# One-hot rows written token by token, and a copy of x moved from GpSimd to a DMA of SyncE

## What is computed

```python
# 1. attention in windows: chunks of 32 queries, 16 keys to the left, 8 to the right, 8 memory keys
# 2. experts
skip_score = x @ w_skip
do_compute = skip_score > 0
out = x.copy()
xc = x[do_compute]
logits = xc @ w_gate                       # 8 experts
e_idx = np.argmax(logits, axis=1)
gate_w = softmax(logits)[.., e_idx]
for e in range(E):
    mask = e_idx == e
    h = np.maximum(xc[mask] @ w1[e], 0.0)  # 512 -> 1024
    y[mask] = gate_w[mask, None] * (h @ w2[e])
out[do_compute] = xc + y
# 3. h = max(x @ w1, x @ w2, x @ w3); result = h @ w_out
```

## Time and profile before

| | us |
|---|---|
| three runs: median | 673.62 |
| lowest, highest | 672.19, 688.42 |
| the profiled execution's own time | 675.65 |
| its span, first to last instruction | 673.9 |
| PE busy in the span | 651.8 (97%) |
| DVE / ACT / POOL busy | 460.1 / 318.9 / 174.6 |
| granted TensorE clock, mean | 1.000 of full |

### The profile page before, as it was taken

One profiled execution on the slowest core, in us unless ns is written; L12 is line 12 of the kernel. 1 busy time (PEld: TensorE's weight loads), 2 busy tenths in 40 slices (PEclk: granted clock), 3 DMA queues, 4 the chain that ended last, 5 costly groups with the idle time before them and its releaser, 6 DMA issues.

```text
span 673.9 us, 13069 instructions
## 1 busy us (share of the span) xinstructions
PE 651.8 (97%) x4864; PEld 542.4 (80%) x4864; DVE 460.1 (68%) x820; ACT 318.9 (47%) x504; POOL 174.6 (26%) x210
## 2 busy tenths in 40 slices
PE   4999989999999999999999999999999999999998
PEld 3778865788997999988888888888888888888886
DVE  4778867877666656798899873378889516888500
ACT  4445442556544555564455453345456424445311
POOL 7411222476675375405300012100000220000000
DMA  8999964767675587713601115121101111110011
GB/s 301 410 328 341 344 232 175 262 233 265 199 245 166 180 298 248 234 41 119 214 32 63 62 48 188 47 64 62 63 32 63 59 67 52 44 63 32 0 63 62
DMA packets 32505, 101.07 MB, mean 150 GB/s; under 512 B 6012, under 2 KB 6156, under 8 KB 32336
## 3 DMA queue, kind: packets, MB, share of 16 engines
q1 hardware_dynamic: 26288, 87.12, 37.6%
q0 software_dynamic: 6176, 13.41, 5.7%
HBM read 87.11 MB, written 16.80 MB: 154 GB/s over the span
## 4 chain that ended last, share of the span: by engine, by line
PE 89%; DVE 4%; DMA 2%; issue 2%; ACT 1%; another core or an unknown queue 1%; SPq 1%; DVEq 0%; ACTq 0%
PE ps_c L1620 9%; PE ps_c L1622 9%; PE ps_c L1621 8%; PE ps_b L1622 5%; PE ps_b L1620 5%; PE ps_b L1621 5%; PE ps_s L1490 4%; PE ps_h L1620 4%; PE ps_h L1622 4%; PE ps_h L1621 4%; PE ps_o L1505 4%; PE ps_y L1620 3%; PE ps_y L1621 3%; PE ps_y L1622 3%; PE ps_f L1622 2%; PE ps_f L1620 2%
## 5 line engine op out<-in xcount | busy, mean ns | idle before, releaser
L1215 DVE TENSOR_TENSOR w_lo<-raw,w_hi 128x1024 fp32r<-128x1024 f32 x64 | 79.5, 1254 | 42.1 <-ACT w_hi L837 33.7
L837 ACT ACTIVATE w_hi<-raw 128x1024 fp32r<-128x1024 f32 x64 | 67.8, 1060 | 47.6 <-PE ps_y L1622 26.2
L1238 DVE TENSOR_TENSOR u_lo<-u_f,u_hi 128x1792 fp32r<-128x1792 f32 x27 | 54.6, 2023 | 50.3 <-ACT u_hi L826 50.3
L1620 PE MATMUL ps_c<-c_hi,u_lo 128*128 128x512 f32 x216 | 85.2, 394 | 0.6
L1622 PE MATMUL ps_c<-c_hi,u_hi 128*128 128x512 f32 x216 | 84.2, 390 | 0.0
L1621 PE MATMUL ps_c<-c_lo,u_hi 128*128 128x512 f32 x216 | 84.2, 390 | 0.0
L1620 PE MATMUL ps_h<-x_hi,w_lo 128*128 128x256 f32 (+1 forms) x256 | 71.5, 279 | 1.7 <-DVE w_lo L1215 0.9
L1622 PE MATMUL ps_h<-x_hi,w_hi 128*128 128x256 f32 (+1 forms) x256 | 71.9, 281 | 0.0
L1621 PE MATMUL ps_h<-x_lo,w_hi 128*128 128x256 f32 (+1 forms) x256 | 71.9, 281 | 0.0
L777 POOL DMA_INDIRECT out<-f_out,order x16 | 17.6, 1100 | 207.5 <-ACT f_out L792 206.9
L792 ACT ACTIVATE f_u<-ps_c 128x512 f32<-128x512 f32 x58 | 34.6, 597 | 69.8 <-PE ps_c L1622 67.5
(11 more groups left out here) (240 smaller groups left out, 1504.3 us busy)
## 6 DMA issues: line engine op xcount, KB each, us to landing
raw<-wpack SPq DMA_DIRECT2D x64, 512.0 KB
u_f<-wunit SPq DMA_DIRECT2D x27, 512.0 KB, 3.3
v_sb<-vW SPq DMA_DIRECT2D x32, 390.0 KB, 5.3
k_sb<-kT SPq DMA_DIRECT2D x32, 250.0 KB, 4.9
q_sb<-qT SPq DMA_DIRECT2D x16, 384.0 KB, 6.0
x_dram<-x_buf SPq DMA_DIRECT2D x4, 1536.0 KB, 10.2
f_in<-x_dram SPq DMA_DIRECT2D x1, 2048.0 KB, 9.0
out<-f_out SPq DMA_DIRECT2D x8, 256.0 KB, 2.0
```

The source lines that it names most:

```text
L837: act.activation(w_hi[c % RING][:, :], raw[:, c % RAW, :], ACT.Copy).then_inc(s_whi, 1)
L1215: dve.tensor_tensor(w_lo[c % RING][:, :], raw[:, c % RAW, :], w_hi[c % RING][:, :].bitcast(F32), ALU.subtract).then_inc(s_wlo, 1)
L1238: dve.tensor_tensor(u_lo[n % UBUF][:, 1:8, :], u_f[n % UBUF][:, 1:8, :], u_hi[n % 2][:, :, :].bitcast(F32), ALU.subtract).then_inc(s_ulo, 1)
L1620: pe.matmul(out_, a_lo, b_hi, start=first, stop=False, skip_group_check=goes_on)
```

## The change

`oh_row` is laid out token by token: `[P, NTT, P]`, so that the 128 numbers which PE loads for one column lie next to each other. It is written by 24 instructions in place of four: each compares the numbers 0 to 127 (`iota`, now stored once, not six times) with one number per partition, `row[:, t:t + 1]`, which is float32 instead of bfloat16. PE waits before each of its 24 products instead of before every sixth.

The copy of `x_in` to `x_nat` leaves GpSimd. SP starts a DMA for it in every pass (`keep_rows`), between the weight chunks 5 and 6, after it has waited for the gathered rows and for the sums of the pass before. GpSimd's next gather into `x_in` and DVE's sums wait for that DMA (`s_xnat`).

```diff
-            iota = sb("iota", [P, P, ROWS], BF16)
+            iota = sb("iota", [P, P], BF16)
-            row = sb("row", [P, NTT], BF16)
-            oh_row = sb("oh_row", [P, NTT // ROWS, P, ROWS], BF16)
+            row = sb("row", [P, NTT])
+            oh_row = sb("oh_row", [P, NTT, P], BF16)
...
+            def keep_rows(i):
+                for t in range(TB):
+                    sp.wait_ge(s_gath[t], i * 16 + 16)
+                sp.wait_ge(s_xo, i * TB + TB)
+                sp.dma_start(x_nat[:, :, :], x_in[:, :, :]).then_inc(s_xnat, 16)
+
+            def load_rest(e, i):
+                for c in range(LEAD, FB):
+                    load_chunk(e, c, i * FB + c + 1)
+                    if c == 5:
+                        keep_rows(i)
...
-                pool.iota(iota[:, :, :], pattern=[[1, P], [0, ROWS]], base=0, channel_multiplier=0,
+                pool.iota(iota[:, :], pattern=[[1, P]], base=0, channel_multiplier=0,
...
-            def take_rows(i):
-                pool.wait_ge(s_xo, i * TB + TB)
-                order_()
-                pool.tensor_copy(x_nat[:, :, :], x_in[:, :, :]).then_inc(s_nat, 1)
-
             def next_rows(i):
                 pool.wait_ge(s_tr, i + 1)
-                pool.wait_ge(s_nat, i * 2 + 1)
+                pool.wait_ge(s_xnat, i * 16 + 16)
                 pool.wait_ge(s_idx, i + 1)
...
-            for n in range(NTT // ROWS):
-                dve.tensor_tensor(oh_row[:, n, :, :], iota[:, :, :],
-                                  row[:, n * ROWS:(n + 1) * ROWS].unsqueeze(1).to_broadcast([P, P, ROWS]), ALU.is_equal)\
-                    .then_inc(s_row, 1)
+            for t in range(NTT):
+                dve.tensor_scalar(oh_row[:, t, :], iota[:, :], row[:, t:t + 1], None, ALU.is_equal).then_inc(s_row, 1)
...
             def sums_out(i, tokens):
-                dve.wait_ge(s_nat, i * 2 + 2)
+                dve.wait_ge(s_xnat, i * 16 + 16)
+                dve.wait_ge(s_nat, i + 1)
                 dve.wait_ge(s_landed, i + 1)
...
             for t in range(NTT):
-                n, j = t // ROWS, t % ROWS
-                if j == 0:
-                    pe.wait_ge(s_row, n + 1)
-                last = pe.matmul(spots, oh_row[:, n, :, j], val[:, :, :, t].rearrange("p v n -> p (v n)"),
+                pe.wait_ge(s_row, t + 1)
+                last = pe.matmul(spots, oh_row[:, t, :], val[:, :, :, t].rearrange("p v n -> p (v n)"),
                                  start=False, stop=(t == NTT - 1))
```

More of the change, by code:

```diff
@@ L77 @@
 B12, B11, B22, B21, T1, T2, T3, T4 = range(8)
-ROWS = 6
 NIX = 2
@@ L368, in build @@
         s_nat = sem("s_nat")
+        s_xnat = sem("s_xnat")
         s_h = sem("s_h")
@@ L496, in load_pass @@
                 e_next = sp.value_load(table[0:1, bass.ds(i + 1, 1)], min_val=0, max_val=E - 1)
-                for c in range(LEAD, FB):
-                    load_chunk(e_now, c, i * FB + c + 1)
+                load_rest(e_now, i)
                 for c in range(LEAD):
@@ L509, in _ @@
             e_last = sp.value_load(table[0:1, bass.ds(last, 1)], min_val=0, max_val=E - 1)
-            for c in range(LEAD, FB):
-                load_chunk(e_last, c, last * FB + c + 1)
+            load_rest(e_last, last)
             for n in range(2, UBUF):
@@ L681, in next_gates @@
                 pool.tensor_copy(idx_q[:, :], gidx[:, bass.ds(i * TB + TB, TB)]).then_inc(s_idxq, 1)
-                pool.wait_ge(s_nat, i * 2 + 2)
+                pool.wait_ge(s_nat, i + 1)
                 pool.wait_ge(s_idxq, i + 2)
@@ L718, in begin @@
             def begin(i):
-                take_rows(i)
                 next_rows(i)
@@ L724, in begin @@
                 rows_there(i - 1)
-            for t in range(TB):
-                pool.wait_ge(s_gath[t], 16)
-            take_rows(0)
             next_rows(0)
```

## The result

| | before | after |
|---|---|---|
| median of 22 runs each, us | 673.59 | 676.22 |
| lowest, highest | 671.83, 688.42 | 673.05, 679.43 |
| the profiled execution | 675.65 | 679.01 |
| its span | 673.9 | 676.9 |

The changed kernel is slower by 0.41%: ratio 1.0041, 95% interval [1.0028, 1.0054].

What follows compares the result with a forecast made beforehand. PE, busy 97% of the span, was taken to bound the kernel. One-hot rows +1.0 us and the x copy off GpSimd -1.1 us summed to -0.1 us: 673.5 us from the median 673.62, range 671.0 to 677.0.

Steps and rivals of the forecast that it cites:

- DVE's rate: Routing, one-hot rows: 24 DVE instructions start 0.20 us apart and become PE's clock, so `idx_f` comes 1.0 us later.
- The bounds of 0.13 and 0.27: Routing: limits for DVE's row spacing in us, putting `idx_f` between 0.6 us earlier and 2.7 us later.
- The middle: Routing: the chosen row spacing of 0.20 us between those limits, the rate of the instruction replaced.
- Rival 1: Routing: DVE rows cheaper, 0.16 us apart, costing +0.2 us; sum -0.9, total 672.7 us; chance 25%.
- The 20 added waits of PE lie within DVE's 0.20.: Routing, PE's 24 products: the extra waits add nothing beyond DVE's 0.20 us per row.
- The copy off GpSimd, -1.1 us: Pass 1: without GpSimd's copy the `w_lo` pair ends 1.2 us earlier and PE regains 0.9 to 1.2 us.
- SP's queue and the DMA engines: Start of passes: the x copy's DMA fits SP's spare 3 us and largely idle DMA engines; cost nothing.
- the hole: Pass 1, 142 to 144 us: DMA engines almost idle (0.05 and 0.00), where the x copy would largely fall.
- my upper bound of 6.1: The 512 KB x copy by DMA: bounded between 3.3 and 6.1 us.
- GpSimd's chain ... Both still fit ... Nothing.: Passes 0 and 1: gather 1.6 to 4.4 us later, yet `g_nat` and `rows_there` still in time; cost nothing.
- Rival 3: Passes 0 and 1: x copy delays chunk 6 or 7 by over 1 us; +1.9, 675.5 us; chance 18%.
- rival 4: Pass 3: ACT's unexplained 2.98 us pause goes or another comes, giving 670.8 or 676.3 us; chance 10%.

Runs made afterwards that it cites:

- experiment 1: Kernel before with only the new one-hot rows (`oh_row`), GpSimd still copying x: 677.15 us, ratio 1.0022.
- 4: Kernel before with the new one-hot rows and PE reading its two loop bounds ahead of the 24 products: 674.71 us, ratio 1.0011.
- experiment 14: Kernel before with GpSimd gathering the gates of pass 0 before it takes the rows: 673.88 us, ratio 0.9996.
- experiment 12: Kernel before plus an unused 512 KB SBUF-to-SBUF DMA per pass but the last, in SP's queue where the change copies x: 674.28 us, ratio 1.0006.
- 13: Changed kernel with PE's two reads ahead of the 24 products and GpSimd gathering pass 0's gates before waiting for the copy: 673.18 us, ratio 0.9978.
- 5: Changed kernel with the x copy of pass 0 started behind weight chunk 3 instead of chunk 5: 675.4 us, ratio 1.0014.
- 8: Changed kernel with GpSimd gathering the gates of pass 0 before it waits for the x copy: 677.23 us, ratio 1.0029.
- experiment 15: Changed kernel, unedited, profiled a second time: 674.01 us.
- experiment 3: Changed kernel with PE reading its two loop bounds before the 24 products instead of after them: 679.23 us, ratio 1.0052.

## Why the prediction was wrong

The time moved by +0.41% where the sum gave -0.1 us. By its own steps:

- **DVE's rate.** The step took 0.20 us a row and `idx_f` +1.0 us. Measured: 0.163 us and +0.2 us. The bounds of 0.13 and 0.27 held it. The middle was too high: either the number per partition and the width don't cost one after the other as I had added them, or the width costs less in this form; the runs don't tell the two apart. By the Trainium skill ("VectorE: DVE Perf Modes", section on the perf-mode tier table) `tensor_scalar` on bfloat16 in SBUF runs at twice the rate of `tensor_tensor`; with the fixed part from the earlier trace rows that gives, as an estimate, starts 0.16 us apart, and the trace agrees with its 0.163. Rival 1 had this step right.
- **"The 20 added waits of PE lie within DVE's 0.20."** This step failed first. They do, each for itself; but I counted the waits and not what stands behind the last. Before, the last row was done at 111.97, 2.0 us before the filling began at 113.96, and the reads fitted in between, or so the absence of any gap says; now the last row is done at 113.83, the reads come after it, and PE stands still for 1.22 us. Experiments 1 and 4 show it by taking the reads away. By itself the pause would have cost little, since before PE waited 1.33 us for the first rows anyway; nor did slow filling products by themselves, as experiment 14 shows. The two together, a start 1.6 us later and 1.7 us more of filling, are more than that slack: the rows landed 0.8 us later, PE turned them 1.0 us after that, and less the 0.25 us that it used to wait for `x_lo` this is the +1.5 us to the first product. That the pause made the clock fall isn't shown. All six profiles with the pause have slow filling products (5.96 to 7.36 us), but so have three of the five with the new rows and the reads ahead (5.55, 5.61 and 6.18), and one of the seven with the old rows (experiment 14).
- **The copy off GpSimd, -1.1 us.** Near in size, but partly by luck in place. In the changed kernel the pair of `w_lo` takes 2.35 us and PE's pause is gone, as said. But that pause belongs to the one execution before that I had read. Of the other four with GpSimd's copy, experiment 1 has a pair of 2.99 us and a pause of 0.37, and 4, 12 and 14 have 2.35 to 2.42 and no pause. There the copy held up DVE in pass 0 instead: `u_f` took 1.14 and 1.26 us (4, 12) in place of 0.42, and `moved` 1.79 (14), where 4 has 0.19. So most of the 1.55 us that 13 wins in pass 1 is not the copy's: 4, with the copy on GpSimd, has a pass 1 of 17.77, and 13 has 17.68. The nearest pair is 4 and 13, both with the new rows and the reads ahead: 13 is 0.8 us shorter up to the end of pass 1, nearly all of it before the first product, and the two ratios, on two chips, are apart (1.0011 [0.9999, 1.0023] and 0.9978 [0.9962, 0.9995]).
- **SP's queue and the DMA engines.** The copy didn't fall into the hole alone but in pass 0 behind three chunks, and took 6.45 us, just beyond my upper bound of 6.1. The traffic itself costs nothing that can be measured (experiment 12), as the step said.
- **"GpSimd's chain ... Both still fit ... Nothing."** The second failure, and the larger one. The shift was forecast well: gather at 125.0 to 127.8 (measured 127.79), gates later by 1.6 to 4.4 us. I then checked two of the things that hang on the chain, `g_nat` and `rows_there`. `g_nat` came 6.6 us later, since each gather on the way took up to 1.1 us longer; it cost 0.4 us in pass 0. I didn't check the third, the gather of pass 1, against PE's turn of the rows in step 6 of that pass. It moved from the hole at 142 to 144 us into the busiest stretch of the DMA engines, and PE waited 3.9 us for it, or ACT for chunks. Experiments 5 and 8 show it from two sides: either one brings the gather back to about 145.5, and the waits are gone in its profile. Rival 3 had the place (GpSimd's chain, the chunks) and near the size (675.5), at 18%, but a chunk late by over 1 us, which it wanted, is in only one of the three profiles (experiment 15).
- **The pause in pass 3** went away, rival 4's good end, and this hid 2.9 us of the loss in the profile. (Its 2.98 us on either side of 673.5 give 670.5 and 676.5, not the 670.8 and 676.3 written there; nothing hangs on it.) Pauses of 1 to 3 us without a cause that the trace shows stand in passes 2 to 4 of several kernels, the kernel before among them, and in others not.

What stays open: what makes the clock fall during the filling products; why the half clock holds for 20 us and more in some executions once it is there; what ends up late in pass 1 of a given execution; and whether the pauses of passes 2 to 4 have to do with any of these edits.

## What to carry to other kernels

When a step is made later, follow its queue to the end: list everything that stands behind the new wait on the same engine, register reads included, and for each the time at which somebody needs it, one pass further than seems necessary. A copy handed to a DMA cost next to nothing here in bytes and a lot in place: it paid only after the waiter behind it had been given other work first. Mends don't add up by themselves: 3 and 5 together were no better than the change, 3 and 8 took its whole loss back. And a pause that one trace shows can lie elsewhere in the next execution: before it is put into a sum, look whether a second execution has it too.

## What the runs showed of the hardware

- A DVE compare of 128 bfloat16 numbers per partition with one float32 number per partition takes 247 to 251 ns, but the next can start 0.163 us after it.
- A weight load of 128 x 128 bfloat16 takes 96 ns with the numbers side by side and 125 ns at a stride of 12 bytes.
- A DMA of 512 KB within SBUF lands after 2.9 to 3.3 us at the median, as fast as a load of that size from DRAM (3.3 us), and after 6.45 us behind three such loads.
- Two reads of a register from SBUF cost PE 1.21 to 1.25 us when it has to sit them out (six profiles).
- Beside a GpSimd copy of 1.04 to 1.20 us a DVE `tensor_tensor` takes longer: `u_f` 1.14 and 1.26 us in place of 0.42, the pair of `w_lo` 3.55 in place of 2.35.
- After 1.2 us of idle PE, in the middle of small products, the granted clock was 0.50 for some 3 us; in experiment 14 it was 0.50 from 114 to 116 with no such pause. After waits of 2.09 and 1.77 us in pass 1 it was 0.56 to 0.59 for 4 us; in experiment 3, after a wait of 0.92 us, 0.50 for 25 us; before, after a wait of 0.93 us, it stayed at 1.00.
